# A delta-rule attention and two expert layers on one core: the second set-up around the first state, fewer wide products ahead of the first solve, POOL's values behind the scaling, the low parts split

## The reference

```python
# q, k, v: (4, 8, 768, 48), beta: (4, 8, 768)
k_n = k / (norm(k) + 1e-6)
for t in range(S):                       # delta rule, state is (B, H, 48, 48)
    y[t] = q[t] @ state
    v_old = k_n[t] @ state
    state = state + beta[t] * outer(k_n[t], v[t] - v_old)
x = y.reshape(3072, 384)
x = ((x @ w1) * (x @ w2)) @ w3 @ w_out   # d_ff = 1024
logits = x @ phi                         # 32 slots = 8 experts x 4
d = softmax over the tokens; slot_in = d.T @ x
slot_out[e] = relu(slot_in[e] @ e1[e]) @ e2[e]
out = softmax over the slots (logits) @ slot_out
```

## Time and profile before

| | us |
|---|---|
| median of three runs | 541.73 |
| lowest, highest | 541.46, 551.67 |
| profiled execution | 544.47 |
| its span, first to last instruction | 542.7 |
| PE busy | 486.4 (90%) |
| POOL busy | 185.1 (34%) |
| DVE busy | 244.0 (45%) |

### The profile page before, as it was taken

How to read it: one execution, slowest core, us unless ns; L and a number is a source line. 1 busy time by engine, 2 the same in 40 slices (tenths; PEclk the granted TensorE clock), 3 DMA queues, 4 the chain that set the end, 5 groups by cost and what they waited for, 6 DMA issues and landing times.

```text
span 542.7 us, 24391 instructions
## 1 busy us (share of the span) xinstructions
PE 486.4 (90%) x11300; PEld 349.3 (64%) x11300; DVE 244.0 (45%) x536; ACT 140.9 (26%) x277; POOL 185.1 (34%) x334
## 2 busy tenths in 40 slices
PE   5768898959999899998999998999999999779964
PEld 5354566747777677776777776777777777324433
DVE  2998484156442455324453354623523321524423
ACT  0223322212322232222322222222222222113313
POOL 1002088830688006880058810588100000000000
PEclk9878999969999999999999999999999999599997
DMA  8995000800004500036000260000430608986928
GB/s 215 367 317 239 4 4 6 232 4 4 4 2 100 138 5 4 2 83 156 5 4 2 69 171 4 5 2 4 184 133 4 234 6 321 413 311 236 356 107 348
DMA packets 28437, 65.15 MB, mean 120 GB/s; under 512 B 1968, under 2 KB 15408, under 8 KB 28080
## 3 DMA queue, kind: packets, MB, share of 16 engines
q1 hardware_dynamic: 27888, 62.81, 34.6%
q10 hardware_dynamic: 448, 0.79, 0.6%
HBM read 58.87 MB, written 4.72 MB: 117 GB/s over the span
## 4 chain that ended last, share of the span: by engine, by line
PE 76%; POOL 7%; DMA 4%; SPq 4%; issue 4%; DVE 3%; ACT 1%; DVEq 0%; POOLq 0%
PE pB L1108 18%; PE pA L1108 16%; POOL prep_slab L437 4%; PE pD L1048 4%; PE pK L1030 3%; PE pY L1061 3%; POOL prod_p L436 3%; PE pK L1008 3%; DMA arena<-kq_dram 2%; PE pT L1124 2%; PE pG L1124 2%; PE pD L1132 2%; PE pY L1015 2%; SPq L317 2%; PE pT L990 2%
## 5 line engine op out<-in xcount | busy, mean ns | idle before, releaser
L436 POOL TENSOR_TENSOR prod_p<-prep_slab 128x30 f32<-128x30 f32 (+9 forms) x150 | 74.5, 497 | 51.8 <-DVE prep_slab L700 40.8
L634 DVE TENSOR_TENSOR arena<-a_sb,pB 128x512 f32<-128x512 f32 x42 | 28.9, 688 | 140.6 <-PE pB L1108 140.5
L437 POOL TENSOR_TENSOR prep_slab<-prep_slab,prod_p 128x30 f32<-128x30 f32 (+9 forms) x150 | 82.6, 551 | 11.7
L1108 PE MATMUL pB<-whi,xhi 128*128 128x512 f32 x138 | 59.5, 431 | 0.0
L1108 PE MATMUL pB<-whi,xlo 128*128 128x512 f32 x138 | 54.6, 396 | 0.0
L1108 PE MATMUL pB<-wlo,xhi 128*128 128x512 f32 x138 | 54.5, 395 | 0.0
L1108 PE MATMUL pA<-whi,xlo 128*128 128x512 f32 x138 | 49.4, 407 | 4.7 <-DVE xlo L629 4.7
L1108 PE MATMUL pA<-whi,xhi 128*128 128x512 f32 x138 | 51.0, 422 | 1.2 <-issue 1.2
L1108 PE MATMUL pA<-wlo,xhi 128*128 128x512 f32 x138 | 47.0, 395 | 0.0
L476 ACT ACTIVATE a_sb<-pA 128x512 f32<-128x512 f32 x48 | 28.8, 600 | 61.0 <-PE pA L1108 60.8
L429 POOL TENSOR_SCALAR_AFFINE_SELECT prep_slab<-prep_slab 128x1024 f32<-128x1024 f32 x5 | 6.3, 1265 | 90.1 <-DVE sys_s L668 90.1
(11 more groups left out here) (246 smaller groups left out, 834.2 us busy)
## 6 DMA issues: line engine op xcount, KB each, us to landing
late_w<-e_dram SPq DMA_DIRECT2D x8, 1536.0 KB, 9.6
arena<-kq_dram SPq DMA_DIRECT2D x44, 192.0 KB, 5.6
arena<-e_dram SPq DMA_DIRECT2D x5, 1536.0 KB, 11.5
arena<-kv_dram SPq DMA_DIRECT2D x16, 384.0 KB, 6.0
out_dram<-late_w SPq DMA_DIRECT2D x6, 768.0 KB, 4.9
arena<-w3t_dram SPq DMA_DIRECT2D x2, 2048.0 KB, 19.6
arena<-w_dram SPq DMA_DIRECT2D x1, 4096.0 KB, 14.0
arena<-kv_dram SPq DMA_DIRECT2D x2, 1536.0 KB, 20.3
```

Of the source, the lines that this page charges most:

```text
L436: link(nc.gpsimd.tensor_tensor(pv, a, x, ALU.mult))
L437: link(nc.gpsimd.tensor_tensor(dst, dst, pv, ALU.add))
L634: nc.vector.tensor_tensor(ab_tile(s, p)[:, half * HF:(half + 1) * HF], a_sb[:], pB[:], ALU.mult).then_inc(ab_done, 1)
L1108: last = mm((pA, pB)[w][:], lhs[:, c * 128:(c + 1) * 128], rhs[:, w, c, fc], start=(k == 0), stop=(k == 3 * KC - 1))
```

## The change

Seven edits, all in what comes before and in iteration 0:

1. PE: of the nine products with 384 columns the last two stay (28 and 29); ahead of them stand a wait for p_done and 27 small products like those at the start. The wait for p_done behind them goes.
2. DVE, step 0: set_up_root(1) comes ahead of the state, and set_up_rest(1) behind it.
3. DVE, steps 0 and 1: the masks of iteration 0's steps 1 to 3 move from behind the state of step 0 to behind the right-hand side of step 1, where set_up_root(1) and set_up_rest(1) stood.
4. DVE, step 2: w_low(1, 1) moves behind the product ab_mul of the first half.
5. DVE, step 2: the masks of iteration 1 move from ahead of w_low to the end of the step.
6. POOL: for iteration 1 the values of steps 1 to 3 wait until DVE has scaled that iteration's X and copied its diagonal.
7. The small products at the start become a function (no other order).

```diff
-AWAKE = range(21, 30)
+SMALL, AWAKE = 27, (28, 29)
...
                     link(nc.gpsimd.tensor_tensor(dst, dst, pv, ALU.add))
+                if n == 1:
+                    pool.wait_ge(x_link, 2 * n + 2)
                 values(1, STEPS)
...
                     if g == 0:
                         first_pt(0, 0, 1)
                         set_up(1, q, k)
+                        set_up_root(1)
                         state(g)
-                        first_pt(0, 1, STEPS)
+                        set_up_rest(1, q, k)
                         continue
...
                     r_rows(g, p, s, n)
                     if g == 1:
-                        set_up_root(1)
-                        set_up_rest(1, q, k)
+                        first_pt(0, 1, STEPS)
                     if g == 2:
-                        first_pt(1, 0, STEPS)
                         w_low(1, 0)
-                        w_low(1, 1)
...
                     ab_mul(t, ts, 0, tp)
                     if g == 1:
                         w_low(0, 0)
+                    if g == 2:
+                        w_low(1, 1)
                     mask_at(3)
                     state(g)
...
                     ab_mul(t, ts, 1, tp)
+                    if g == 2:
+                        first_pt(1, 0, STEPS)
...
-            for i in range(FILLERS):
-                q = slice(32 * (i % 4), 32 * (i % 4) + 32)
-                mm(pY[q, 0:32], ident[q, q], ident[q, q], start=True, stop=True)
+            def small_products(count):
+                for i in range(count):
+                    q = slice(32 * (i % 4), 32 * (i % 4) + 32)
+                    mm(pY[q, 0:32], ident[q, q], ident[q, q], start=True, stop=True)
+
+            small_products(FILLERS)
...
             for s in range(STEPS):
                 gram_products(1, s, first_gram[1][s])
+            pe.wait_ge(p_done, 1)
+            small_products(SMALL)
             for k_ in AWAKE:
                 pe.wait_ge(prep_link, X_LINK + 2 * k_)
                 mm(pK[:, 0:DM], ident[:], Macc[:, 0:DM], start=True, stop=True)
             for sem_, i in ((r_done, 1), (x_link, 1), (x_link, 1)):
                 pe.wait_ge(sem_, i)
                 mm(pK[:], ident[:], Macc[:, 0:HF], start=True, stop=True)
-            pe.wait_ge(p_done, 1)
```

## The result

The changed kernel takes 537.79 us (median of 20 runs, 533.56 to 542.46); the kernel before, measured beside it, 542.26 (20 runs). The ratio is 0.9919, with a 95% interval of [0.9892, 0.9946]: 0.8%, some 4.4 us, clear of noise but under the 2% that counts as a change. 12.5 us were forecast. The profiled execution took 538.18, not 532.0; its span is 536.4, 6.3 shorter.

A forecast was written before the change was run, and what follows sets the result against it. PE held 76% of the chain, POOL 7%, with waits before 130 us. PE's restart 9.95 us earlier plus 2.6 of clock gave 12.5 us off the 541.73 base: 529.2 us, range 525 to 534.5, forecast chance 0.45.

The forecast's parts named there:

- the first part's result: PE ahead of the first solve: fewer wide products let it start at 50.2, not 54.0, 3.8 us earlier.
- the sum: PE's restart at the xlo products comes at 105.7, 9.95 us earlier, plus 2.6 from a held clock: 12.5 us.
- the clock stays low: Rival: PE's clock stays low behind the small products, first solve at 53.2; 8.4 us gained, 533.3 us; chance 0.22 with milder form.
- The milder form: Low clock returning to full among the three full-width products, solve at 52: 11.1 us gained, 530.6 us; chance 0.12.
- The clock falls once more at the restart: Rival: PE pauses for its own instructions ahead of the xlo products; 9.95 us gained, 531.8 us; chance 0.12.
- the set-up's move: DVE's second set-up around the first state: POOL starts at 58.4, not 68.2, 9.8 us earlier, less any state product lateness.
- POOL's chain beside DVE: POOL's solve of the second system: 41.7 us plus 0.5 for the moved masks, ending at 100.7.
- the copy: DVE's diagonal copy takes 0.20 instead of 2.00 us once POOL's later values wait: 1.8 us gained.
- the split: Step 2's six low-part subtractions on DVE, three ahead and three behind the product: PE's wait goes, 1.5 us gained.
- the masks: Iteration 0's masks, moved behind step 1's right-hand side on DVE, add 0.5 us to POOL's chain (bounds 0 and 0.95).
- The set-up's move is hidden: Rival: an unseen wait keeps steps 1 to 3 in place but for 4 to 6 us; 536 to 537 us; chance 0.09.
- slower through a low clock in steps 1 to 3: Rival: without wide products PE stays at 1.2 GHz through steps 1 to 3; 554 us if until 113; chance 0.02.

The follow-up runs named there:

- e3: The changed kernel with 16 small products ahead of the wide ones instead of 27; 531.51 us, ratio 0.98 to the kernel before.
- e5: The changed kernel with 36 instead of 47 small products at the very start, the later 27 kept; 537.24 us, ratio 0.9892 to the kernel before.
- e2: The kernel before with PE's edit alone (27 small products, two wide ones instead of nine); 549.69 us, four runs too uneven for a ratio.
- e4: The changed kernel with the second load of keys and values (1.5 MB) issued behind the first solve; 536.15 us, ratio 0.9888 to the kernel before.
- e10: The changed kernel with 24 small products ahead of the wide ones instead of 27; 534.84 us, ratio 0.9798 to the kernel before.
- e12: The changed kernel with 8 small products ahead of the wide ones instead of 27; 532.95 us, ratio 0.9718 to the kernel before.
- e9: As e3, but the second set-up behind step 1's right-hand side and the masks behind the state, as before; 538.97 us, ratio 0.9868 to the kernel before.
- e8: As e3, but step 2's low parts in one piece and iteration 1's masks ahead of them, as before; 535.59 us, ratio 0.9866 to the kernel before.
- e7: As e3, but POOL's later values of iteration 1 don't wait for the scaling; 532.03 us, ratio 0.9821 to the kernel before.
- e6: The changed kernel with no small products ahead of the two wide ones; 536.9 us, ratio 0.9896 to the kernel before.
- e1: The changed kernel without PE's edit: nine wide products as before, all DVE and POOL edits kept; 536.35 us, ratio 0.9892 to the kernel before.

## Why the prediction was wrong

**The step that failed** is the first part's result, "the solve starts at 50.2, not 54.0". It priced a small product by its duration, 0.032 us, and took PE's supply of instructions for granted. The miss of 5.15 us divides about so: at the stall's begin PE was 0.1 late; the stall took 3.56; the last two small products 0.25; the two wide and the three full-width ones took 55.35 - 49.07 = 6.28 where 5.0 were set down. e3, where the border lies elsewhere, has no stall and starts the solve at 48.83.

Behind it the sum fails once more at the same point. It brought PE to the xlo products at 105.7; PE came at 111.64, 5.9 late: the 5.15 from the solve and 1.65 of low clock (below) are 6.8, and 0.9 the other way isn't assigned. PE's stalls between solve and restart are about as much in both kernels (2.94; before 0.62, 0.23, 0.69 and 1.24), so the forecast held them without naming them. From there to L1130 it took 9.25 us, not 10.1. So step 4's state came 7.5 earlier where 12.5 were set down.

**The rival "the clock stays low"** (533.3 us) had the wrong mechanism for the larger part, but its observation was right: the clock was 0.50 beyond 48. That costs 1.3 us of the 5.15, the 6.28 for 5.0. The stall isn't needed for it: in e5, without a stall behind the small products, the wide and full-width ones took 6.66 us. What goes with it is the number of small products: with 27 or 24 (changed, e2, e4, e5, e10) the clock came back at 51.4 to 53.6, with 16 or fewer (seven kernels) at 46.3 to 47.2. The Trainium skill's rule that the gate follows how busy PE has lately been (TensorE: Matmul & The Clock Gate, Part 1, What's actually happening) fits the changed kernel: 1.26 us busy in the 3 us of 44 to 47 and a clock of 0.50 behind it. It doesn't tell of the stall. (The milder form's 530.6 has a slip: by its own working PE, not DVE, is last, at 107.5, which gives 10.8 gained and 531.0.)

**"The clock falls once more at the restart"** had a chance of 0.12, and its cause, a pause of PE for its own instructions, did occur, 2.94 us until 107.86. It took 1.65 us: from the stall's end to the xlo products 3.78 us (107.86 to 111.64), in e3 at the full clock 2.13 (102.10 to 104.23). Whether it falls there differs by kernel (e3 not, e12 for some 10 us, e9 for 13.6), so a chance of 0.12 was low and 2.6 us no bound.

**Right by the runs:** the set-up's move (POOL 5.9 earlier in e3 than in e9; 9.8 was forecast against the kernel before, 10.3 in e3; in the changed kernel 5.8, which is the forecast's own "one less for each microsecond" with the state product 4.1 late), POOL's chain beside DVE (41.9 for 42.3), the copy (1.80 of 1.8, shown in the trace only), the split (forecast 1.5, wait 1.52 before, none now, 2.02 in e8), the masks without a cost that shows. **"The set-up's move is hidden"** named 536 to 537 us, the nearest to 537.79, by "a wait that I don't see". That is in part what happened, and 0.09 was low for it. The waits are PE's stalls, steps 1 and 2 stay where they were (the low parts of x at 76.17 and 91.38, before 75.72 and 91.79), and of the 7.4 us by which the next low part came earlier PE's restart used 4.0. **Not seen:** "slower through a low clock in steps 1 to 3"; the clock held, 1.00 from 53.6 to 108.2.

**From 12.5 to 4.4.** 5.0 are missing by step 4's state, as above. Behind it the changed kernel's profiled execution took 415.4 us, the one before 414.2, e3's 414.9, e10's 410.4, with PE's same code from there on: single executions differ there by some us. So the 3 us between the 7.5 and the ratio's 4.4, of which 1.2 are lost behind step 4 and 1.9 lie between the trace's 6.3 and the 4.4, aren't assigned to an edit.

## What to carry to other kernels

Count instructions, not only durations, on an engine that runs many short ones: four for an fp32 product here, 256 to a block, a block about 3 us behind the last border in quiet and up to 7 in these cases beside bulk transfers. 64 products that last less than that end in a stall, and an edit that adds or removes instructions moves every border behind it, also into places that it doesn't touch (e5). A count of filler work is therefore tuned by a scan of several numbers, with an eye on "issue" in the rows, before its idea is dropped or kept. And the end of the changed stretch is read too: here the low part of x was ready 3.4 us before PE came to it.

## What the runs showed of the hardware

A block of 256 PE instructions was there 2.8 to 3.5 us after the border before it without other transfers (2.8 in e7, e8 and e9, 3.2 to 3.3 before and in e3, e6 and e12, 3.5 in e1), after 5.1 in e4, 6.2 in the changed kernel and in e10, 6.5 in e2 beside loads of up to 445 GB/s, and 7.0 at the changed kernel's restart beside 309. What differs is when its packet starts: 0.7 us behind the border in e3, 3.6 in the changed kernel, 1.1 us long in both. The long stalls for it were 1.4 to 3.96 us, and the profile names them only "issue". A POOL product of 1152 columns held DVE's copy of 32 columns for 2.00 us instead of 0.20 (e7, e3), while the transpose beside it was as fast as in later iterations (1.91 to 2.04, there 1.99 to 2.02).
